# Three of eight experts' weights are split during the first expert pairs instead of during attention

## What is computed

```python
# attention, per position t
C = f_stab * C + i_stab * outer(v[t], k[t]);  n = f_stab * n + i_stab * k[t]
y[t] = sigmoid(o_gate[t]) * (C @ q[t]) / max(|n . q[t]|, 1)
# experts: x is y as [3072, 320]
e = argmax(x @ w_gate);  g = softmax(x @ w_gate)[e]
out = g * (relu(x @ w1[e]) @ w2[e])        # w1[e] 320x1024, w2[e] 1024x320
# dense
h = out @ w_in;  result = max(0.01 * h, h) @ w_out   # 320x2048, 2048x320
```

## Time and profile before

| | before |
|---|---|
| median of 3 runs | 907.21 us |
| the profiled execution | 906.79 us, of it a span of 905.0 us |
| attention, about | 28 to 272 us of the span |
| routing | 272 to 300 us |
| expert pairs | 300 to 530 us |
| dense layer | 530 to 905 us |
| PE busy | 763.7 us, 84% of the span |
| DVE busy | 569.4 us, 63% |
| ACT busy | 361.5 us, 40% |
| transfers | 99.55 MB, mean 110 GB/s |

### The profile page before, as it was taken

How to read it: one execution, slowest core, us unless ns; L and a number is a source line. 1 busy time by engine, 2 the same in 40 slices (tenths; PEclk the granted TensorE clock), 3 DMA queues, 4 the chain that set the end, 5 groups by cost and what they waited for, 6 DMA issues and landing times.

```text
span 905.0 us, 17468 instructions
## 1 busy us (share of the span) xinstructions
PE 763.7 (84%) x6405; PEld 554.4 (61%) x6406; DVE 569.4 (63%) x1536; ACT 361.5 (40%) x647; POOL 157.0 (17%) x192
## 2 busy tenths in 40 slices
PE   0776877776781799999999989999999999999994
PEld 0665765665671687888888875555555555555552
DVE  7677787779788765657776564545545455454341
ACT  2355655655445125325322223343343433433432
POOL 4133343334331111111111000010010010100101
PEclk9999989999895799999999999999999999999997
DMA  4899999996820259333313000000000000000000
GB/s 113 214 255 293 258 323 322 264 307 214 245 97 14 88 178 355 107 114 138 137 31 130 15 3 0 1 15 15 1 30 1 0 29 0 29 0 0 30 1 29
DMA packets 49772, 99.55 MB, mean 110 GB/s; under 512 B 7694, under 2 KB 38094, under 8 KB 46638
## 3 DMA queue, kind: packets, MB, share of 16 engines
q1 hardware_dynamic: 47070, 89.74, 32.0%
q0 software_dynamic: 2640, 9.01, 3.0%
HBM read 74.85 MB, written 23.89 MB: 109 GB/s over the span
## 4 chain that ended last, share of the span: by engine, by line
PE 63%; DVE 17%; issue 10%; ACT 5%; DMA 3%; SPq 1%; POOL 0%; DVEq 0%; ACTq 0%
PE bank L1390 25%; PE bank L1514 13%; PE bank L1424 10%; PE bank L1298 4%; PE bank L1273 3%; DMA slotA<-d_wA 2%; ACT stage L757 2%; DVE qk L1212 2%; DVE slotA L891 1%; PE bank L1282 1%; DVE sxt L1187 1%; ACT stage L774 1%; PE bank L1311 1%; PE bank L1380 1%; PE bank L1290 1%
## 5 line engine op out<-in xcount | busy, mean ns | idle before, releaser
L1390 PE MATMUL bank<-stage,slotA 128*128 128x512 f16 x768 | 181.3, 379 | 0.0
L1514 PE MATMUL bank<-slotB,dec 128*128 128x320 f16 x768 | 159.4, 299 | 15.6 <-DVE qk L1212 13.0
L1207 DVE TENSOR_TENSOR stage<-bank,stage 128x512 f32<-128x512 f32 x96 | 66.3, 691 | 105.4 <-ACT stage L757 105.3
L1390 PE MATMUL bank<-qbd,slotA 128*128 128x128 f16 x1984 | 117.8, 221 | 6.0 <-DVE qbd L1124 3.5
L1390 PEld LDWEIGHTS bank<-qbd,slotA 128*128 128x128 f16 x1984 | 114.9, 99 | 9.4 <-issue 5.4
L1390 PEld LDWEIGHTS bank<-stage,slotA 128*128 128x128 f16 x768 | 75.1, 98 | 74.1
L1514 PE MATMUL bank<-slotB,qk 128*128 128x320 f16 x384 | 114.8, 299 | 0.0
L1514 PEld LDWEIGHTS bank<-slotB,dec 128*128 128x128 f16 x768 | 73.0, 98 | 66.7 <-DVE qk L1212 23.6
L757 ACT ACTIVATE stage<-bank 128x512 f32<-128x512 f32 x96 | 57.4, 598 | 129.1 <-PE bank L1390 129.1
L1424 PE MATMUL bank<-slotB,emov 128*128 128x320 f16 x496 | 102.1, 300 | 4.7 <-issue 3.0
L715 ACT ACTIVATE emov<-bank 128x512 f16<-128x512 f32 x62 | 37.0, 597 | 160.3 <-PE bank L1390 160.3
(11 more groups left out here) (231 smaller groups left out, 1217.1 us busy)
## 6 DMA issues: line engine op xcount, KB each, us to landing
stage<-wB SPq DMA_DIRECT2D x10, 1280.0 KB, 8.1
stage<-wA SPq DMA_DIRECT2D x10, 1024.0 KB, 6.5
slotA<-d_wA SPq DMA_DIRECT2D x6, 1280.0 KB, 6.2
slotB<-d_wB SPq DMA_DIRECT2D x6, 1280.0 KB, 5.8
d_wA<-slotA SPq DMA_DIRECT2D x5, 1280.0 KB, 10.1
d_wB<-slotB SPq DMA_DIRECT2D x5, 1280.0 KB, 6.3
stage<-wA SPq DMA_DIRECT2D x20, 256.0 KB, 8.0
qk<-qkT SPq DMA_DIRECT2D x12, 360.0 KB
```

The lines of the kernel that those rows point to most:

```text
L1207: v.tensor_tensor(fgl[f % 2], bank[f % 2][:, :], ft[f % 2], ALU.max).then_inc(f_g, 1)
L1390: ins = t_.matmul(pf, a[:, col:col + P], x(k), start=(q == 0), stop=(q == len(ops) - 1))
L1514: ins = t_.matmul(bank[4 + q][:, 0:DM], x[f % 2][:, q * P:(q + 1) * P], slotB[2 + f // NF][:, c0:c0 + DM], start=(f == 0 and z == 0), stop ...
```

## The change

Units are now named by expert (8 and 9 are the dense halves) and taken from tables: the order of loads and squares `LOADS`, the order of splits `SPLITS`, the slot, and the half of `stage`. Squares and scales of all eight experts stay in attention. Only the first five splits (`NSPL` = 5: experts 3, 4, 2, 0, 1) stay there. Expert 7 is loaded once for its squares and again for its split. The high parts of 5 and 6 are written by ACT right after attention, those of 7 in pairs 4 and 5. The low parts of 5, 6 and 7 are written by DVE in the pairs, by the table `LOWS`. Stores of 5, 6, 7 and loads of 7, 8, 9 are issued by ACT, in `dense(p)` at p = 3, 5 and 6, six DMAs each time. SP keeps the expert loads and waits for each expert's store first. Squares, scale, high and low parts of the dense halves start at pairs 9, 15, 16 and 17. In attention the logits copy stands ahead of the low part of the third head group.

```diff
+            def load_unit(x):
+                h = SPLIT_HALF[x]
+                m = wA[ds(row(x), 1)].rearrange("a k f -> (a k) f")
+                act.dma_start(stA[h][:, 0:2 * FE].rearrange("p (k f) -> p k f", k=2),
...
+                for r in range(2):
+                    act.dma_start(stA[h][r * KR:(r + 1) * KR, 2 * FE:3 * FE], m[2 * P:DM, :]).then_inc(stgA_landed[h], 16)
+                act.dma_start(stB[h].rearrange("p (n d) -> p n d", n=NF),
...
+            def store_unit(x):
+                act.dma_start(d_wA[row(x)], slotA[SLOT[x]][:, :]).then_inc(stored[x], 16)
+                act.dma_start(d_wB[row(x)], slotB[SLOT[x]][:, :]).then_inc(stored[x], 16)
...
             def dense(p):
+                if p in SPLIT_END:
+                    x = SPLIT_END[p]
+                    act.wait_ge(lo_done, NSL * (split_at(x) + 1))
+                    store_unit(x)
+                    load_unit(x + 2)
+                if p in LAST_HIGH:
+                    for k in LAST_HIGH[p]:
+                        if k == 0:
+                            act.wait_ge(stored[5], 32)
+                            act.wait_ge(stgA_landed[0], 48 * 5)
+                        if k == 3:
+                            act.wait_ge(stgB_landed[0], 16 * 5)
+                        high(NE - 1, k)
...
-            for k in range(NSL):
-                high(NE - 1, slot(NE - 1), k)
+            for x in SPLITS[NSPL:NSPL + 2]:
+                for k in range(NSL):
+                    high(x, k)
...
+                    if g == 2 and st >= 2:
+                        top(st - 2)
                     lows(st, g)
-                if not (is_st(st, 0) or is_st(st, 1)):
-                    top(st - 2)
...
-                if p < 3:
-                    low3(p + 2)
+                early(p)
                 dense(p)
...
-SQ_AT, SCALE_AT, HI_AT, LO_AT = 4, 11, 12, 13
+SQ_AT, SCALE_AT, HI_AT, LO_AT = 9, 15, 16, 17
+LOWS = {-2: [(5, 0)], 0: [(5, 1), (5, 2)], 1: [(5, 3)], 2: [(5, 4), (6, 0)], 3: [(6, 1)], 4: [(6, 2), (6, 3)],
+        5: [(6, 4), (7, 0)], 6: [(7, 1), (7, 2), (7, 3), (7, 4)]}
+SPLIT_END = {3: 5, 5: 6, 6: 7}
+LAST_HIGH = {4: (0, 1), 5: (2, 3, 4)}
+LOADS = (3, 4, 2, 0, 1, 7, 5, 6, 8, 9)
+NSPL = 5
```

More of the change, by code:

```diff
@@ L185, in build @@
         hi_done, lo_done = sem("hi_done"), sem("lo_done")
-        storedA = [sem(f"storedA{i}") for i in range(4)]
-        storedB = [sem(f"storedB{i}") for i in range(4)]
+        stored = [None, None] + [sem(f"stored{x}") for x in range(2, NE)]
         rt = sem("rt")
@@ L440, in _ @@
                 store_x(st, st % NBUF)
[L443 to L449, removed]
-                sp.wait_ge(storedA[i], 16 * (2 if i < 2 else 1))
-                sp.wait_ge(storedB[i], 16 * (2 if i < 2 else 1))
             sp.wait_ge(rt_tab, 1)
@@ L454, in _ @@
                 last = sp.value_load(tab_last[0:1, e - 2:e - 1], min_val=0, max_val=NPAIR)
+                sp.wait_ge(stored[e], 32)
                 sp.wait_ge(m_h, 2 * (last + 1))
@@ L721, in dense @@
                     if j == 0:
-                        act.wait_ge(storedA[3], 16)
-                        act.wait_ge(storedB[3], 16)
+                        for x in (6, 7):
+                            act.wait_ge(stored[x], 32)
                     for q in range(j, j + 2):
@@ L873, in scale_tail, with low @@
                 v.reciprocal(wsc[:, ds(u, 1), :], winv[:, ds(u, 1), :]).then_inc(sc_chain, 1)
-            def low(u, t, k):
-                dve.wait_ge(hi_done, NSL * u + k + 1)
-                x = part(u % 2, k)
+            def low(y, k):
+                dve.wait_ge(hi_done, NSL * split_at(y) + k + 1)
+                x = part(SPLIT_HALF[y], k)
+                t = SLOT[y]
                 if k < 2:
@@ L944, in lows @@
                 u, r = st // UP, st % UP
-                if r == 2 and u < NE - 1:
-                    low(u, slot(u), g)
-                if r == 0 and u > 0 and g < 2:
-                    low(u - 1, slot(u - 1), 3 + g)
+                if r == 2 and u < NSPL:
+                    low(LOADS[u], g)
+                if r == 0 and 0 < u <= NSPL and g < 2:
+                    low(LOADS[u - 1], 3 + g)
             def step(c, b, st):
@@ L1145, in y_add, with early @@
                                        ALU.mult, ALU.add).then_inc(m_y, 1)
-            def low3(k):
-                low(NE - 1, slot(NE - 1), k)
+            def early(p):
+                for y, k in LOWS.get(p, ()):
+                    low(y, k)
             x_scale(0, 0)
-            low3(0)
+            early(-2)
             x_low(0, 0)
```

125 lines of the change are left out of this document (64 added, 61 removed).

## The result

The changed kernel takes **919.57 us** (median of 4 runs, 916.81 to 920.79) against 907.22 us: a ratio of 1.0131, 95% interval 1.0091 to 1.0172. It is slower by 1.3%, 12 us, where I had forecast 902.5 us.

A forecast was written before the change was run, and what follows sets the result against it. PE was taken to bound the pairs, DVE was busiest in routing, and no single engine bound attention. Attention -22 us and pairs +17.7 us gave -4.3 us: 902.5 us against 906.8; own range 896 to 909, with rivals 888 to 914.

The forecast's parts named there:

- Attention: Attention: steps 16 to 21 without two experts' high and low parts, -16.9 us, plus the logits copy, -5 us: -22 us together.
- the 7.05 us that I had read from step 23: Attention, steps 17, 18, 20 and 21: PE's floor for a step without split work, 7.05 us.
- The copy: Attention, steps 2, 5, 8, 11, 14: logits copy ahead of the third low part, 1.0 us each, -5 us, bounds 0 and -6.4.
- Pair 4: Pair 4: ACT waits for expert 5's store and the load of 7's A; PE stalls 4.5 us, bounds 3 and 9.
- Pairs 5 and 6: ACT waits for DVE's low parts, then six issues at 4 us: stalls 6.8 us (2.8 to 13) and 7.1 us (3.1 to 13.5).
- The clock: Pairs: stalls may lower PE's granted clock, and only the slow h behind the last costs: +1 us, bounds 0 and 4.
- the wait for expert 2's A: Pair 7: expert 2's A no longer stands behind the dense loads, -1.7 us.
- issues hold ACT: Rival, pairs: six issues on ACT take 10.4 us as on SP's full queue, net +9.5 us, 916 us; chance 0.13.
- Hidden stalls: Rival, pairs: issues cost next to nothing and loads run at 355 GB/s or more, net -16 us, 891 us; chance 0.27.
- attention held by transfers: Rival, attention: transfers hold steps at 8.7 us, so attention gives only -15 us, net +3, 909 us; chance 0.10.

The follow-up runs named there:

- the spread version: Changed kernel with the late splitting, stores, loads and dense-half work spread over more pairs, each wait referring to work done a pair earlier: 886.03 us.
- the spread ones: Changed kernel with late work spread over the pairs (886.03 us), that with the logits copy put back (890.35 us), and one spread further by its tables (889.74 us).

## Why the prediction was wrong, point by point

**Attention was right in its sum.** Steps 16 to 21 gave -17.97 us (forecast -16.9, bounds -18 and -10): the steps 17 and 20, which I had put at 7.2 us, took 6.86, and step 19 took 7.18 instead of 7.83, while 18 and 21 took 7.62 instead of 7.5. So the 7.05 us that I had read from step 23 are no floor of PE. The transfers did not hold them: the DMA share was 0.76. In all, attention gave -21.8 us, forecast -22, in part by luck, as the next point shows.

**The copy was right in place and half as large in the steps.** At step 2's transpose PE's wait fell from 2.77 us to 1.43 us, the 1.3 us forecast. The copy now stands ahead of the low part:

```profile
59.02 0.15 DVE L958 COPY lgs<-bank 128x8 f32<-128x8 f32 x1
59.20 1.28 DVE L910 SCALAR_TENSOR_TENSOR slotA<-stage,wsc,slotA 64x1024 f16<-64x1024 f32 x1
```

```profile
59.27 0.51 PE L1330 MATMUL bank<-ident,og 128*120 128x128 f32 x3 [1.43 <-issue]
```

But the step got 0.70 us of it and the next gave 0.17 back: 0.53 us a step, not 1.0. Five steps are 2.7 us; the forecast was 5. Steps 1 to 15 together still went from 154.1 to 150.2 us, because in the kernel before steps 5 and 8 took 11.33 us where the same code in the spread version with the old copy took 10.60; the window from 120 to 130 us had a granted clock of 0.66 there. Attention met its sum because the copy's shortfall, these 1.5 us of the clock, and 1.1 us more than forecast in steps 16 to 21 nearly cancelled; that the sum met the forecast to 0.2 us is luck.

**Pair 4 failed, at its upper bound.** The step was: ahead of the landing lie 5.5 MB, landing 17 us after the first issue, stall 4.5 us. Measured: 22.9 us and 9.0 us. (The stall grew by less than the landing, because the issues began 11.5 us ahead of h(5) and not 10.0.) The mechanism was right. Wrong were mainly the bytes, since expert 2's B, which SP issues 11 us after ACT's first issue from its own queue, shares the engines, and 0.33 MB of gathers do too: 7.1 MB instead of 5.5. The test with that B later took 3.9 us off the stall. The pace was near: 339 GB/s from 309 to 330 us, not 355, with about 2 us around it for which the lower bound had nothing. (That bound is 328.7 + 15.5 = 344.2, not 345 as the prediction writes; the stall of 3 us goes with 344.2.) The fit of one DMA in the Trainium skill ("DMA: Bandwidth & Descriptors", Anatomy of one DMA) gave 14.6 us as an estimate; the trace, with 22.9 us, does not agree. The page states it for one DMA of the software path, and these were several in two queues. The measurement decides.

**Pairs 5 and 6 failed in the price of the issues.** With the issues on SP the stalls were 3.2 and 4.0 us; my waits for the low parts and high parts, 6.8 - 4 and 7.1 - 4, are 2.8 and 3.1, nearly that. The term of 4 us for six issues measured 6.2 and 6.4 us. I took it from the argument that the queue is empty at first. In pair 3 that held: six issues in 3.3 us. In pair 5 it held for the first two (0.34 and 0.46 us); but the stores began to move, and the loads behind them cost 5.3 us instead of 2.2. I had named 6.2 us as the point from which the change loses. It was just reached; what pair 4 and the clock lost on top made the change clearly slower. With the issues on SP the kernel takes 901.5 us instead of 919.6, of which 12.5 us are the issue time in pairs 5 and 6, 3.9 us the order of expert 2's B, and 1.9 us the slow interval behind h(8). The Trainium skill ("DMA: Bandwidth & Descriptors", Issuing engines are not separate DMA queues) has the rule that issuing from a second engine saves only issue time. The runs agree that no bandwidth came with ACT's queue: from the first issue to the landing in pair 4 the windows show 330 GB/s with two queues and 337 with SP's alone.

**The clock cost more than I had allowed.** Windows of the kernel after: the stall of pair 4, the product behind it, and h(8).

```profile
332.00:336.00 4.00, 0.00 (x0) 0.00 (x0) 2.07 (x4) 2.75 (x5) 0.00 (x0) 0.50 0.45 153
336.00:342.00 6.00, 5.71 (x54) 5.71 (x55) 4.64 (x13) 0.00 (x0) 0.94 (x1) 0.50 0.23 82
370.00:377.00 7.00, 6.12 (x65) 6.13 (x66) 3.42 (x13) 0.60 (x1) 0.94 (x1) 0.56 1.00 375
```

With PE idle the granted clock is 0.50 (1.2 GHz), and it stays there through h(6). As I had said, that is paid mainly behind the last stall: h(8) to h(9) took 9.70 us, +2.3 instead of +1. Not foreseen was a slow h(1), 5.33 us instead of 3.74, which with what follows it costs 2.1 us between h(0) and h(2). Of the seven kernels with the pairs of this change six have it, and neither the spread ones nor those with the old pairs; the code up to there is the same as in the spread ones, and why the clock rises sooner in some is open.

**The sum.** Attention -21.8; slow clock at h(1) and other small losses up to h(2) +2.1, and +0.8 up to h(5); stalls 9.0 + 9.4 + 10.3 = +28.7; the wait for expert 2's A -1.7 (as forecast: h(7) waits for no DMA); the clock behind h(8) +2.3. Together +10.4 us; measured +10.0. Against my sum of -4.3 that is 14.7 us: 10.3 in the three stalls (4.5, 2.6 and 3.2), 2.9 ahead of them, 1.3 in the clock behind them, and 0.2 in attention.

**The rivals.** Nearest came the slower one, "issues hold ACT", 916 us, to which I gave 0.13. Its price of 10.4 us for six was too high, but its mechanism is the largest single part of the loss: 12.5 us. Without it, and without the slow interval that goes with it, about 905 us would be left, which these runs cannot tell from no change; the 901.5 us with the issues on SP hold the 3.9 us of the other order as well. "Hidden stalls" fell because the waits for low parts and landings stand whatever an issue costs, "attention held by transfers" because the DMA share fell to 0.76. The range ended at 914, since I had let the bounds of three stalls and of the clock fall one by one and not together, though one cause, a queue busy with the moved transfers, pushes all of them the same way.

## What to carry to other kernels

Moving work off a transfer-bound stage pays only if the place it goes to never makes a compute engine wait in line for it: ask of each wait in the new place whether what it waits for was finished a stage earlier, and give each stage one small piece. An engine that converts for the bottleneck should not issue large DMAs in a burst: it pays for the issues, and more once its queue is moving. For a landing, count the bytes that the other queues move until then, and those ahead in the own queue, but not those behind, and add what the trace shows of time before the first packet and after the last.

## What was not expected of the hardware

- The time to issue a DMA on ACT was not fixed. The same four loads: 2.2 us with ACT's queue at rest, 5.3 us while its stores move; one store's issue took 6.65 us behind the transfers of the pair before, and two behind four loads took 5.6 us.
- The queues of SP and ACT share the DMA engines, 330 GB/s together against 337 from SP's alone, but not evenly: of what these two moved from 323 to 330 us, 1.31 MB were SP's and 0.57 MB ACT's. 1.3 MB in the other queue cost 3.5 us of landing, 1.3 MB later in the own queue nothing.
- Steps of the same code took 0.7 to 1.2 us longer where the granted clock was 0.66 to 0.84, at other steps in each kernel; one took 1.5 us longer (step 13 with expert 2's B later, 11.75 us) in a window of 0.90. Such steps move by some microseconds what any two kernels differ by; 3 us of difference in attention with the same code is one example.
